# Last list of tiles in units of 128 rows, two units of any two experts to a tile

## The reference, cut to what matters

```python
w = np.exp(weight_gen - weight_gen.max(-1, keepdims=True)); w /= w.sum(-1, keepdims=True) + 1e-9
out = np.einsum('bshk,bskhg->bshg', w, x_unf)        # 4 x 3584 rows of 192, 8 heads, 7 taps
```

```python
noisy = x @ w_gate + np.log1p(np.exp(x @ w_noise)) * noise
top2 = np.argpartition(-noisy, 2, axis=1)[:, :2]     # and a softmax over the two
for e in range(8):
    for k in range(2):
        mask = top2[:, k] == e
        h = np.maximum(x[mask] @ w1[e], 0.0)         # 192 -> 1024
        out[mask] += top2_w[mask, k, None] * (h @ w2[e])   # 1024 -> 192
```

## Time and profile before

| | us |
|---|---|
| median of 3 runs | 1219.96 (1219.89 to 1221.6) |
| the profiled execution | 1221.09 |
| its span, first to last instruction | 1219.3 |
| TensorE busy | 1145.7 (94%) |
| VectorE busy | 864.8 (71%) |
| ScalarE busy | 661.0 (54%) |
| GpSimd busy | 680.3 (56%) |
| granted TensorE clock, mean share | 0.975 |

### The profile page before, as it was taken

One profiled execution on the slowest core, in us unless ns is written; L12 is line 12 of the kernel. 1 busy time (PEld: TensorE's weight loads), 2 busy tenths in 40 slices (PEclk: granted clock), 3 DMA queues, 4 the chain that ended last, 5 costly groups with the idle time before them and its releaser, 6 DMA issues.

```text
span 1219.3 us, 35682 instructions
## 1 busy us (share of the span) xinstructions
PE 1145.7 (94%) x12139; PEld 1043.7 (86%) x12139; DVE 864.8 (71%) x1738; ACT 661.0 (54%) x1120; POOL 680.3 (56%) x494
## 2 busy tenths in 40 slices
PE   5765699999999999999999999999999999999996
PEld 2332498999999999999999999999999999999996
DVE  6889488796969969697896969879696543333332
ACT  6864554647465474655547465565645544444442
POOL 1045356485765848567584766748576664333343
PEclk9787799999999999999999999999999999999998
DMA  9997425344353444435344343443534463333322
GB/s 301 271 326 212 131 49 134 54 109 83 66 126 68 110 86 101 92 65 128 67 107 94 63 120 69 115 82 86 108 56 83 68 147 55 49 48 51 45 25 24
DMA packets 110638, 124.22 MB, mean 102 GB/s; under 512 B 11383, under 2 KB 102799, under 8 KB 108814
## 3 DMA queue, kind: packets, MB, share of 16 engines
q0 software_dynamic: 45024, 46.59, 24.5%
q1 hardware_dynamic: 65454, 75.34, 21.6%
HBM read 62.24 MB, written 59.63 MB: 100 GB/s over the span
## 4 chain that ended last, share of the span: by engine, by line
PE 86%; ACT 4%; POOL 3%; DVE 2%; issue 2%; DMA 2%; SPq 0%; ACTq 0%; DVEq 0%; PEldq 0%; POOLq 0%
PE psum L1106 13%; PE psum L1108 13%; PE psum L1109 13%; PE psum L1093 8%; PE psum L1089 8%; PE psum L1090 8%; PE psum L1091 8%; PE psum L1092 8%; POOL sorted_rows L388 3%; PE psum L1078 3%; PE psum L1039 1%; PE psum L1018 1%; DMA sorted_rows<-rows,pos 1%; ACT rows L482 1%; PE psum L1049 1%
## 5 line engine op out<-in xcount | busy, mean ns | idle before, releaser
L399 POOL DMA_INDIRECT out_rows<-late,st x238 | 390.5, 1641 | 382.0 <-ACT late L523 218.7
L884 DVE SCALAR_TENSOR_TENSOR hidden<-psum,hidden 128x512 f16<-128x512 f32 x476 | 327.3, 688 | 289.1 <-ACT hidden L512 284.6
L512 ACT ACTIVATE hidden<-psum 128x512 f16<-128x512 f32 x476 | 283.9, 597 | 438.9 <-PE psum L1093 438.2
L1106 PE MATMUL psum<-w2s,hidden 128*128 x1904 | 468.4, 246 | 4.7 <-ACT late L523 4.7
L1108 PE MATMUL psum<-w2s,hidden 128*128 x1904 | 468.4, 246 | 0.0
L1109 PE MATMUL psum<-w2s,hidden 128*128 x1904 | 468.3, 246 | 0.0
L1089 PE MATMUL psum<-xT,w1s 128*128 128x256 f16 x952 | 260.2, 273 | 1.0 <-ACT xT L508 1.0
L1090 PE MATMUL psum<-xT,w1s 128*128 128x256 f16 x952 | 260.2, 273 | 0.0
L1091 PE MATMUL psum<-xT,w1s 128*128 128x256 f16 x952 | 260.2, 273 | 0.0
L1093 PE MATMUL psum<-xT,w1s 128*128 128x256 f16 x952 | 260.2, 273 | 0.0
L1092 PE MATMUL psum<-xT,w1s 128*128 128x256 f16 x952 | 260.2, 273 | 0.0
(11 more groups left out here) (175 smaller groups left out, 1196.1 us busy)
## 6 DMA issues: line engine op xcount, KB each, us to landing
st<-sorted_rows SPq DMA_DIRECT2D x119, 202.0 KB, 3.8
xb<-in_x SPq DMA_DIRECT2D x12, 1344.0 KB
out_rows<-zeros SPq DMA_DIRECT2D x19, 576.0 KB, 8.7
st<-in_moe_w SPq DMA_DIRECT2D x5, 768.0 KB, 9.8
out_rows<-late,st POOLq DMA_INDIRECT x238
wb<-in_weight_gen SPq DMA_DIRECT2D x14, 224.0 KB, 2.9
w2s<-in_moe_w SPq DMA_DIRECT2D x3, 768.0 KB, 13.3
sorted_rows<-pads SPq DMA_DIRECT2D x9, 202.0 KB, 3.8
```

What stands on the lines that cost most here:

```text
L399: pool.indirect_dma_start(out=out, out_offset=bass.IndirectOffsetOnAxis(ap=xr[t % XB][:, s, D + E:D + E + 1].bitcast(I32), axis=0), in_=yo ...
L512: act.activation(hh[:, 2 * q:2 * q + 2, :].rearrange("p j t -> p (j t)"), psH[q][:, :], ACT.Relu).then_inc(hh_ready, 1)
L884: v.scalar_tensor_tensor(hl[:, hq, :].rearrange("p j t -> p (j t)"), psH[q][:, :], 0.0, hh[:, hq, :].rearrange("p j t -> p (j t)"), ALU.ma ...
L1106: nc.tensor.matmul(o, hh[:, j, hs], hi, start=(j == 0 and s == 0), stop=False, skip_group_check=True)
```

## The change

Full tiles (0 to 96) stay as they are. The last list is laid out in units of 128 rows, HALVES = 37 of them, each with an expert of its own, and two units that follow each other make a tile: PAIRED = 19 tiles, the last with one unit. There are then 116 tiles. In such a tile `up` runs the five matmuls once per unit, with 128 columns each; `down` has the same matmuls with weights by unit; the row load, the offset load and the gate product are made once per unit; and since one row of the output may be in both units, GpSimd waits for the first accumulating scatter to land before it starts the second.

```diff
-TILES = (2 * N + E * (T - 1)) // T
+WHOLE = sure(CHUNKS - 1)
+HALVES = (2 * N - WHOLE * T + E * (P - 1)) // P
+PAIRED = (HALVES + 1) // 2
+TILES = WHOLE + PAIRED
+LAST = HALVES
+TP = WHOLE + LAST
+def columns(t):
+    first = WHOLE + 2 * (t - WHOLE)
+    return (t,) if t < WHOLE else tuple(range(first, min(first + 2, TP)))
+def parts(t):
+    return TH if t < WHOLE else len(columns(t))
...
-                r = sp.value_load(rowt[0:1, t:t + 1], min_val=0, max_val=E * RPE)
-                sp.dma_start(xr[t % XB][:, :, :], xs[bass.ds(r, T), :].rearrange("(s p) w -> p s w", p=P)
-                             ).then_inc(xr_loaded[t % XB], 16)
+                for s, c in enumerate(columns(t)):
+                    r = sp.value_load(rowt[0:1, c:c + 1], min_val=0, max_val=E * RPE)
+                    if t < WHOLE:
...
+                    else:
+                        sp.dma_start(xr[t % XB][:, s, :], xs[bass.ds(r, P), :]).then_inc(xr_loaded[t % XB], 16)
...
-                for s in range(TH):
+                for s in range(parts(t)):
                     pool.wait_ge(yo_ready, t * TH + s + 1)
+                    if s and t >= WHOLE:
+                        pool.wait_ge(added, (t * TH + s) * 16)
                     pool.indirect_dma_start(
...
-                e = dve.value_load(et[0:1, t:t + 1], min_val=0, max_val=E - 1)
...
+                for s, c in enumerate(columns(t)):
+                    e = dve.value_load(et[0:1, c:c + 1], min_val=0, max_val=E - 1)
...
             def up(t, q, o1):
 
+                wide = T if t < WHOLE else P
                 for jj in range(2):
                     j = 2 * q + jj
-                    o = psH[q][:, jj * T:(jj + 1) * T]
-                    col = lambda kind: w1s[:, bass.ds(o1 + (kind * F + j * P), P)]
-                    xa, xbx, xc = (xT[t % 2][:, b, :] for b in range(3))
-                    nc.tensor.matmul(o, col(0), xa, start=True, stop=False)
...
+                    for s, at1 in enumerate(o1):
+                        ts = slice(s * wide, (s + 1) * wide)
+                        o = psH[q][:, jj * T + ts.start:jj * T + ts.stop]
+                        col = lambda kind: w1s[:, bass.ds(at1 + (kind * F + j * P), P)]
+                        xa, xbx, xc = (xT[t % 2][:, b, ts] for b in range(3))
+                        nc.tensor.matmul(o, col(0), xa, start=True, stop=False)
...
-                        hi, lo = (w2s[:, bass.ds(o2 + (2 * j + k) * D, D)] for k in range(2))
+                        hi, lo = (w2s[:, bass.ds(o2[s % len(o2)] + (2 * j + k) * D, D)] for k in range(2))
...
-                o = pe.value_load(off[0:1, t:t + 1], min_val=0, max_val=(E - 1) * F)
-                return o * (W1E // F), o * (W2E // F)
+                o = [pe.value_load(off[0:1, c:c + 1], min_val=0, max_val=(E - 1) * F) for c in columns(t)]
+                return [a * (W1E // F) for a in o], [a * (W2E // F) for a in o]
```

More of the change, by code:

```diff
@@ L85, with loads @@
 SLOT_US = 1.45
+def columns(t):
[3 more added lines that the diff above has]
+    return TH if t < WHOLE else len(columns(t))
+def loads(t):
+    return 16 * sum(len(columns(u)) for u in range(t % XB, t + 1, XB))
 def first_column(n):
@@ L332, in _ @@
                 group, k = t // TPC, t % TPC
-                if t == LAST_FROM:
+                if t == WHOLE:
                     write_pads()
@@ L520, in output_rows @@
                     act.wait_ge(tile_added, t - NB + 1)
-                act.wait_ge(gates_ready, t + 1)
-                for s in range(TH):
+                act.wait_ge(gates_ready, columns(t)[-1] + 1)
+                for s in range(parts(t)):
                     act.activation(yo[buf][:, s, :], psY[:, s * D:(s + 1) * D], ACT.Copy,
@@ L688, in lay_out @@
                 dve.wait_ge(counts_done, n - ALONE + 2)
+                unit = P if final else T
                 if final:
-                    ch.link(v.tensor_scalar(cnt[:, :], psCnt, float(T - 1), None, ALU.add))
+                    ch.link(v.tensor_scalar(done[:, :], done[:, :], float(T // P), None, ALU.mult))
+                    ch.link(v.tensor_scalar(cnt[:, :], psCnt, float(P - 1), None, ALU.add))
                     v.tensor_tensor(padrow[:, :], psCnt, eoff[:, 0, :], ALU.add).then_inc(padrow_ready, 1)
@@ L693, in lay_out @@
                     ch.link(v.tensor_copy(cnt[:, :], psCnt))
-                ch.link(v.tensor_scalar(tilesi[:, :], cnt[:, :], T.bit_length() - 1, None, ALU.logical_shift_right))
+                ch.link(v.tensor_scalar(tilesi[:, :], cnt[:, :], unit.bit_length() - 1, None, ALU.logical_shift_right))
                 ch.link(v.tensor_tensor(rem[:, :], tilesi[:, :], done[:, :], ALU.subtract))
@@ L701, in lay_out @@
                 ch.link(v.tensor_tensor(le[:, j, :], ends[:, 1:].unsqueeze(1).broadcast_to([P, tiles, E]),
-                                        jt[:, j, :], ALU.is_le))
+                                        jt[:, 0, j].unsqueeze(2).broadcast_to([P, tiles, E]), ALU.is_le))
                 ch.link(v.tensor_tensor(delta[:, 0:E - 1], gap[:, 1:], gap[:, 0:E - 1], ALU.subtract))
-                ch.link(v.tensor_scalar(delta[:, 0:E - 1], delta[:, 0:E - 1], float(T), float(RPE), ALU.mult, ALU.add))
+                ch.link(v.tensor_scalar(delta[:, 0:E - 1], delta[:, 0:E - 1], float(unit), float(RPE), ALU.mult, ALU.add))
                 yield 0.6
@@ L709, in lay_out @@
                 ch.link(v.tensor_reduce(base[:, j], lt[:, j, :], AX.X, ALU.add))
-                ch.link(v.tensor_tensor(base[:, j], base[:, j], jrow[:, j], ALU.add))
-                ch.link(v.scalar_tensor_tensor(base[:, j], done[:, 0:1].broadcast_to([P, tiles]), float(T), base[:, j],
+                ch.link(v.scalar_tensor_tensor(base[:, j], jt[:, 0, j], float(unit), base[:, j], ALU.mult, ALU.add))
+                ch.link(v.scalar_tensor_tensor(base[:, j], done[:, 0:1].broadcast_to([P, tiles]), float(unit), base[:, j],
                                                ALU.mult, ALU.add))
@@ L869, in beside_parts @@
                         yield first + AT_NORM, normalise_w(n + 1)
-                yield SHARED * SLOTS + AT_COUNTS + 1, lay_out(CHUNKS, LAST_FROM, LAST, final=True)
+                yield SHARED * SLOTS + AT_COUNTS + 1, lay_out(CHUNKS, WHOLE, LAST, final=True)
             def gates(t):
                 buf, rows_in = t % NB, xr[t % XB]
-                dve.wait_ge(xr_loaded[t % XB], (t // XB + 1) * 16)
-                e = dve.value_load(et[0:1, t:t + 1], min_val=0, max_val=E - 1)
-                v.tensor_tensor(gsel[buf][:, :].unsqueeze(2), rows_in[:, :, bass.ds(e + D, 1)],
-                                cw[:, bass.ds(e, 1)].unsqueeze(1).broadcast_to([P, TH, 1]), ALU.mult
-                                ).then_inc(gates_ready, 1)
+                dve.wait_ge(xr_loaded[t % XB], loads(t))
+                for s, c in enumerate(columns(t)):
+                    e = dve.value_load(et[0:1, c:c + 1], min_val=0, max_val=E - 1)
+                    part = slice(0, TH) if t < WHOLE else slice(s, s + 1)
+                    v.tensor_tensor(gsel[buf][:, part].unsqueeze(2), rows_in[:, part, bass.ds(e + D, 1)],
+                                    cw[:, bass.ds(e, 1)].unsqueeze(1).broadcast_to([P, part.stop - part.start, 1]), ALU.mult
+                                    ).then_inc(gates_ready, 1)
             def low_hidden(t, q):
@@ L1073, in transpose_x @@
             def transpose_x(t):
-                pe.wait_ge(xr_loaded[t % XB], (t // XB + 1) * 16)
+                pe.wait_ge(xr_loaded[t % XB], loads(t))
                 r16 = xr[t % XB][:, :, :].bitcast(F16)
                 for b in range(3):
-                    for s in range(TH):
+                    for s in range(parts(t)):
                         last = nc.tensor.transpose(psX[:, b * T + s * P:b * T + (s + 1) * P],
@@ L1082, in up @@
             def up(t, q, o1):
+                wide = T if t < WHOLE else P
                 for jj in range(2):
                     j = 2 * q + jj
-                    o = psH[q][:, jj * T:(jj + 1) * T]
-                    col = lambda kind: w1s[:, bass.ds(o1 + (kind * F + j * P), P)]
-                    xa, xbx, xc = (xT[t % 2][:, b, :] for b in range(3))
-                    nc.tensor.matmul(o, col(0), xa, start=True, stop=False)
[L1090 to L1093, removed]
+                    for s, at1 in enumerate(o1):
[4 more added lines that the diff above has]
+                        nc.tensor.matmul(o, col(0), xa, start=True, stop=False)
+                        nc.tensor.matmul(o, col(0), xc, start=False, stop=False)
+                        nc.tensor.matmul(o, col(1), xa, start=False, stop=False)
+                        nc.tensor.matmul(o, col(2), xbx, start=False, stop=False)
+                        last = nc.tensor.matmul(o, col(3), xbx, start=False, stop=True)
                 last.then_inc(h_done, 1)
```

16 lines of the change are left out of this document (6 added, 10 removed).

## The result

The changed kernel takes 1290.68 us (median of 4 runs, 1289.41 to 1291.88), the kernel before 1220.78 (4 runs): a ratio of 1.0572, with an interval of 1.0553 to 1.059. The forecast was 1285 us, 6 us short of it, and inside its range. The execution profiled took 1290.62 us, 69.5 more than the one profiled before.

What follows compares the result with a forecast made beforehand. TensorE's array bounds the kernel before, and its sequencer would bound the changed one: 1800 addresses x 0.128 + 37 loads x 0.7 = 256.3 us, ending the span 63.4 us later; 1221.1 + 63.4 = 1284.5, predicted 1285 us, range 1255 to 1308.

Steps and rivals of the forecast that it cites:

- The bound: Last list: TensorE's array limits at 8.66 us a tile before; its sequencer at 13.7 us a tile after.
- The step, 0.128 us: TensorE's sequencer: each address's register instruction takes 0.128 us start to start, 96 a full tile for 48.
- the loads, 0.7 each: TensorE's sequencer: each offset load takes 0.7 us, two per full tile for one, 37 in the count.
- No wait comes on top: Last list: ScalarE and VectorE add no waits to the sequencer's 256.3 us; last matmul ends near 1269.0.
- The start and the end: Start: 0 to -0.3 us from one GpSimd constant less; end: last scatters in series, span over at 1282.7.
- The sum: Whole span: last matmul 60.6 us later, span end 63.4 us later, at 1282.7.
- At nothing: Layout step, second expert load and product on VectorE, and SP's second row load cost nothing, hidden under idle time.
- A: Last list: addresses formed in time, array stays the bound at 8.76 us a tile; 1195 us, faster; chance 9%.
- B: Last list: scatter landings at 4.86 us make GpSimd the bound, 12.8 us a tile; 1267 us; chance 3%.
- C: Up matmuls: 128 columns don't hide a 98 ns weight load, 12.1 us a tile; 1255 us; chance 4%.
- D: Last list: gaps in feeding the array drop its clock to 1.2 GHz, 17.5 us a tile; 1355 us; 4%.

Runs made afterwards that it cites:

- packed_addresses: Changed kernel with byte offsets and up to four address additions per register instruction, 24 instead of 96 per full tile: 1201.36 us, 0.9851; repeated on a third chip 1199.24 us.
- same_address: Changed kernel with both units of a last-list tile using the first unit's expert weights, so 48 address instructions fewer per full tile: 1201.73 us, 0.9852.
- before_packed: Kernel before with packed addresses only, 16 register instructions a tile for 48: 1245.18 us, 0.9843 on the second chip; 1220.17 us, 1.0001 on a third.
- packed_spill: packed_addresses without the wait between a tile's two scatters, second units' rows to another buffer: 1219.57 us, 0.9633 on the second chip; 1195.2 us, 0.9799 on a third.
- down_shared_80: Changed kernel with the first unit's expert for both units in down, 80 addresses per full tile for 96: 1299.24 us, 1.0285 on the second chip.

## Why the prediction was right, and its 6 us

**The bound.** Right. The array set the time before, the sequencer after. Register instructions run with no pause; taking half of them away with the same matmuls gives 89 us back, and adding 16 and an offset load to each tile of the kernel before costs it 26.

**The step, 0.128 us, and the loads, 0.7 each.** Right in kind, a little short in size: 96 x 0.128 + 1.4 is 13.7 us a tile, 14.1 was measured. The forecast's count can be read off term by term in the sequencer's records. From the first of its 1800 addresses (1011.69) to the last (1276.50) it is 264.8 us for 256.3. The addresses take 238.5 of them for 230.4, since their mean step in the new list is 0.132 and not 0.128. The 37 loads take 24.3 for 25.9: they don't overlap, but are 0.66 each. 19 semaphore instructions, which the sum hadn't, take 2.0. The forecast read 0.126 and 0.132 from times given to a tenth of a us; the records of the same stretches have 0.128 and 0.130, so the value it took was right for the kernel before, and the longer steps weigh more in the new list. "No wait comes on top" held but for one: in the last tile, which has one unit, an address comes 0.67 us behind the one ahead, and its matmul waits 0.34 us for VectorE (1276.14). The last matmul ended at 1276.94, not 1269.0.

**The start and the end.** The start was 0.75 us early (tile 97's transposes at 1011.97 for 1012.72). The end was to take 13.7 us from the last matmul to the end of the span and took 11.9. The timeline of GpSimd, start, us, what, and the idle time ahead with its releaser, answers to the earlier trace rows:

```profile
1261.42 1.55 POOL L420 DMA_INDIRECT out_rows<-late,st  x1 [8.21 <-ACT late L544]
1266.10 1.55 POOL L420 DMA_INDIRECT out_rows<-late,st  x1 [3.13 <-DMA out_rows<-late,st]
...
1272.67 1.55 POOL L420 DMA_INDIRECT out_rows<-late,st  x1 [5.01 <-ACT late L544]
...
1276.96 1.55 POOL L420 DMA_INDIRECT out_rows<-late,st  x1 [2.74 <-DMA out_rows<-late,st]
1281.24 1.55 POOL L420 DMA_INDIRECT out_rows<-late,st  x1 [2.73 <-DMA out_rows<-late,st]
```

The steps are 4.29 and 4.28 us for the forecast 4.35, and from the last scatter's end (1282.79) it is 6.0 us to the end of the span for 6.6. Tile 114's first scatter stood 4.3 us ahead of the last matmul's end, for 3.2 in the forecast.

**The sum.** +7.9 at the last matmul and -1.8 behind it are the 6.1 us by which the span, 1288.8, passed the 1282.7 of the forecast.

**At nothing.** Right, as far as the totals tell. The scatter wait is hidden in the list: the timeline has 8.21 and 5.01 us in which GpSimd waited for ScalarE ahead of the first scatter of a tile, and in the waits from 1030 to 1265 us no engine waited for GpSimd. Nor did any wait there for SP's row loads.

**The rivals.** A was the rival on the other side, and packed_addresses is what it described: with the addresses in time the array sets 8.89 us a tile (forecast 8.76) and the kernel is faster than before, at 1199 to 1201 us for A's 1195. The 0.13 us are, by the timeline, a pause ahead of one up matmul in each tile, behind the offset loads, and make 2.4 us in 18 tiles. In the profiled execution the list from tile 97's transposes to the last matmul is 3.2 us longer than A had it, those 2.4 among them; the stretch behind the last matmul (15.0 us) is 4.1 longer than before for A's 2.2; and the start was 1.35 us earlier.

B was not seen in any run. GpSimd's series is as long as the tile in same_address and nearly so in packed_addresses, but no engine waits for it, and most of its waits for a landing in the last list took 2.7 to 3.0 us, the longest 4.5. C is refuted by the 0.056 us above.

D's fall of the clock did come, twice, for 3.4 us each, and changed nothing. The windows around the first, as in the earlier trace rows:

```profile
1083.50:1086.90 3.40, 2.31 (x24) 1.65 (x21) 0.75 (x3) 0.00 (x0) 0.25 (x1) 1.00 0.31 31
1086.90:1090.30 3.40, 3.40 (x28) 3.12 (x28) 0.69 (x1) 0.60 (x1) 0.00 (x0) 0.50 0.26 66
```

TensorE was busy 2.31 of 3.40 us, with the offset loads in that stretch, and its clock then stood at 0.50 (1.2 GHz) for the next 3.4 us; ahead of the second (from 1185.9) it was busy 2.37. The forecast argued from 2.66 of 3.40 with the clock still at 1.00, and that wasn't enough to rule the fall out. No cost shows: the array started 28 matmuls in the stretch at 0.50, for 24 in the one ahead, and the tile around it was 14.09 us, like the others, as the sequencer set it. D as it stood, a clock of 0.5 throughout the list and 1355 us, is refuted by the 0.99.

## What to carry to other kernels

Count the register instructions on TensorE's sequencer and set their count times the distance between their starts (some 0.13 us here) against the array's time: it is a second limit that neither the busy share nor the listed 46 ns shows. A change that makes tiles smaller or mixes weights within a tile leaves the array's work nearly as it was and multiplies the addresses. Before the tiling is given up, make the addresses cheaper: byte offsets that need one addition, and several additions made side by side so that they share an instruction.

## What the runs showed of the hardware beyond that

An instruction that forms one address is listed at 46 ns with three operations and at 32 ns with one, and costs 0.129 and 0.118 us by the tiles' distances. With the additions packed, four to an instruction ahead of the up matmuls, it is still short (by line, packed_addresses, 1100 to 1109 us):

```profile
L1113 PEldq FUSED_REGOPS  x25: 55/55/84, 1100.1 to 1109.0; - x25
```

24 of these serve a tile that needed 96.

The second chip took 1262 us where two others took 1220, with the granted clock at 1.00 from 200 to 1000 us on either, and with the same distance of tiles in the last list. The kernel before was not profiled there; in the three kernels that were, all of the extra time lay ahead of that list, and packed kernels lost less there (tile 97's transposes at 1035 for before_packed, 1038 for packed_spill, 1052.72 for down_shared_80, which isn't packed, and 1010 to 1014 on the first chip). From 200 to 1000 us the waits of down_shared_80 show stalls of up to 2.6 us put down to issue, on TensorE, ScalarE and VectorE; the changed kernel, profiled where the kernel before takes 1220 us, has a third as much on the line where TensorE's are longest:

```profile
PEld psum L1134 <- issue: 21.8, 25, 2.6
```

```profile
PEld psum L1134 <- issue: 6.6, 11, 1.4
```

The first row is down_shared_80's, the second the changed kernel's. Why that chip stalls, and why fewer register instructions help, wasn't tried and stays open.
